# An attention stage rewritten ahead of two feed-forward layers on one core: host-side layout, spans of 38 keys, softmax in PSUM, a new order of stages

## The reference

```python
q_d = q.reshape(B, H, Sd, 4, D).mean(axis=3)      # k_d, v_d likewise; Sd = 144
out_d = sm_attn(q_d, k_d, v_d)                    # full softmax attention over 144 positions
out_up = np.repeat(out_d, 4, axis=2)
mask = np.abs(pos[:, None] - pos[None, :]) < 4    # local attention: 7 keys for each query
scores = np.where(mask, scale * np.matmul(q, k.transpose(0, 1, 3, 2)), -1000000000.0)
attn = softmax(scores); out_local = np.matmul(attn, v)
x = (out_up + out_local) as (B*S, H*D)            # 1152 x 512
h = x @ w_in; x = (h * sigmoid(h)) @ w_out        # w_in 512x2048, w_out 2048x512
p = domain_probs / (domain_probs.sum(-1, keepdims=True) + 1e-09)
out += p[:, e:e+1] * (np.maximum(x @ w1[e], 0.0) @ w2[e])   # 4 experts, each 512x1024x512
```

## Time and profile before

| what | value |
|---|---|
| median of 3 runs | 708.74 us (707.76 to 709.19) |
| the profiled execution: its time, its span | 708.72 us, 706.6 us |
| PE busy | 676.7 us (96%) |
| DVE, ACT, POOL busy | 241.7, 187.9, 173.5 us |
| first score product to the last pair's | 8.0 to 81.2 us |
| first `out1` product | at 103.85 us |

### The profile page before, as it was taken

One profiled execution on the slowest core, in us unless ns is written; L12 is line 12 of the kernel. 1 busy time (PEld: TensorE's weight loads), 2 busy tenths in 40 slices (PEclk: granted clock), 3 DMA queues, 4 the chain that ended last, 5 costly groups with the idle time before them and its releaser, 6 DMA issues.

```text
span 706.6 us, 11146 instructions
## 1 busy us (share of the span) xinstructions
PE 676.7 (96%) x3958; PEld 622.3 (88%) x3958; DVE 241.7 (34%) x376; ACT 187.9 (27%) x399; POOL 173.5 (25%) x121
## 2 busy tenths in 40 slices
PE   6768889999999999999999999999999999999997
PEld 5546679999999999998989899999999998989896
DVE  6988968753222322221221212121212121212211
ACT  4765873322111213343101142111241111101010
POOL 5836467660000004546000063000261000000000
PEclk9986989999999999999999999999999999999999
DMA  9454523430000002324100033000040000001001
GB/s 183 102 107 97 136 77 129 143 116 1 1 1 1 0 0 89 119 90 142 36 0 0 1 120 119 0 0 0 30 148 0 0 0 0 0 0 45 21 23 45
DMA packets 66870, 37.48 MB, mean 53 GB/s; under 512 B 32672, under 2 KB 59552, under 8 KB 66848
## 3 DMA queue, kind: packets, MB, share of 16 engines
q1 hardware_dynamic: 66848, 37.19, 18.7%
HBM read 34.82 MB, written 2.36 MB: 53 GB/s over the span
## 4 chain that ended last, share of the span: by engine, by line
PE 88%; DVE 4%; SPq 3%; issue 2%; DMA 1%; ACT 1%; DVEq 0%; POOL 0%; ACTq 0%; POOLq 0%
PE ps L874 42%; PE ps L940 28%; PE ps L924 14%; SPq L278 2%; DMA k_raw<-k 1%; SPq L258 1%; PE ps L789 1%; PE ps L856 1%; PE ps L777 1%; PE ps L841 1%; DVE g_hi L713 1%; PE ps L885 1%; DVE pl L669 0%; DVE kz L434 0%; DVE mx L643 0%
## 5 line engine op out<-in xcount | busy, mean ns | idle before, releaser
L733 DVE SCALAR_TENSOR_TENSOR g_lo<-ps,g_hi 128x384 fp32r<-128x384 f32 x96 | 53.5, 558 | 270.7 <-ACT g_hi L568 270.7
L568 ACT ACTIVATE g_hi<-ps 128x384 fp32r<-128x384 f32 x96 | 47.1, 491 | 293.5 <-PE ps L874 293.5
L397 POOL TENSOR_TENSOR wa_lo<-w_raw,wa_hi 128x1024 f32 (+1 forms) x24 | 57.4, 2395 | 214.8 <-ACT wa_hi L440 214.8
L874 PE MATMUL ps<-x_hi,wa_hi 128*128 (+1 forms) x288 | 97.6, 339 | 2.2 <-issue 2.2
L874 PE MATMUL ps<-x_hi,wa_lo 128*128 (+1 forms) x288 | 97.4, 338 | 0.0
L874 PE MATMUL ps<-x_lo,wa_hi 128*128 (+1 forms) x288 | 97.2, 338 | 0.0
L874 PE MATMUL ps<-x_hi,wb_hi 128*128 (+1 forms) x288 | 96.9, 336 | 0.0
L874 PE MATMUL ps<-x_lo,wb_hi 128*128 (+1 forms) x288 | 96.9, 336 | 0.0
L874 PE MATMUL ps<-x_hi,wb_lo 128*128 (+1 forms) x288 | 96.8, 336 | 0.0
L397 POOL TENSOR_TENSOR wb_lo<-w_raw,wb_hi 128x1024 f32 x24 | 57.7, 2408 | 106.7 <-ACT wb_hi L440 106.4
L713 DVE CAST g_hi<-g_act 128x384 fp32r<-128x384 f32 x48 | 42.7, 889 | 111.3 <-ACT g_act L563 111.3
(11 more groups left out here) (99 smaller groups left out, 1018.5 us busy)
## 6 DMA issues: line engine op xcount, KB each, us to landing
w_raw<-moe_w SPq DMA_DIRECT2D x64, 256.0 KB, 2.8
w_raw<-moe_w_in SPq DMA_DIRECT2D x16, 256.0 KB, 2.9
w_raw<-moe_w_out SPq DMA_DIRECT2D x16, 256.0 KB, 3.0
q_raw<-q SPq DMA_DIRECT2D x16, 144.0 KB, 3.6
k_raw<-k SPq DMA_DIRECT2D x16, 144.0 KB, 3.7
v_raw<-v SPq DMA_DIRECT2D x8, 288.0 KB
out<-o_acc SPq DMA_DIRECT2D x9, 256.0 KB, 2.0
v_win<-v SPq DMA_DIRECT2D x56, 35.0 KB
```

Source lines behind the costliest of these rows:

```text
L397: pool.tensor_tensor(lo[:, at, :].rearrange("p o n -> p (o n)"), w_raw[:, s, :], hi[:, at, :].rearrange("p o n -> p (o n)").bitcast(F32), ...
L568: act.activation(g_hi[:, f % GB, :], ps[:, HB + f % 4, 0:NB], ACT.Relu).then_inc(relu_done, 1)
L733: dve.scalar_tensor_tensor(out=g_lo[:, f % GB, :], in0=ps[:, HB + f % 4, 0:NB], scalar=0.0, in1=g_hi[:, f % GB, :].bitcast(F32), op0=ALU.m ...
L874: ins = pe.matmul(dst, w[:, f % HALF, c], x[:, kt, at], start=(kt == 0 and i == 0), stop=(kt == KT - 1 and i == 2))
```

## The change

**Layout by the host.** The kernel gets five arrays that the host has only rearranged: qk (for each pair, 128 features by 576 queries and 582 keys, the ends repeated), vw (for each pair, head and group of 32 queries, 48 rows of v), vr (v for the means), w (one contiguous 512 KB block a unit), and the probabilities. SP issues four DMAs a pair (one qk, one v, two windows) where it issued fourteen, and one a weight unit where it issued two. The transposes of q and k and their copies out of PSUM are gone.

**Spans of 38 keys.** GQ goes from 64 to 32 queries, W from 70 to 38 keys: 18 groups. Each head is a product of its own on 64 rows of the array (36 products of 32x38 instead of 9 of 64x140); the scores of a partition are 380 elements instead of 700. The values are 36 products of 64x32 instead of 18 of 64x64, and the probabilities of both heads share a transpose (5 instead of 10).

**Softmax in PSUM.** Mask, maximum, subtraction, exponential and sum work in place on two PSUM banks; only the last multiplication writes SBUF. There is one such pair of banks, so a pair's scores wait until the pair before has been multiplied (`pe.wait_ge(pl_ready, n)`).

**Order of stages.** A pair's scores, softmax and mean softmax are in one step, its transposes one step later, its values two steps later; ten steps in all, written out without a loop, instead of eleven with one. DVE normalises the mean softmax (was ACT), ACT computes its bias (was DVE). ACT does `x_high` and `split_hi` last in a step. x_hi and x_lo of pairs 4 to 7 come after the first weight units. EARLY changes from steps 1, 2, 8, 10 to 1, 2, 3, 8.

```diff
-GQ = 64
+GQ = 32
+HS = 64
+ROWS = 48
-        EARLY = {1: 0, 2: 1, N: 2, N + 2: 3}
+        EARLY = {1: 0, 2: 1, 3: 2, N: 3}
...
+            def load_qk(n):
+                if n >= 2:
+                    sp.wait_ge(s_full, n - 1)
+                    sp.wait_ge(qkd_ready, 2 * n - 2)
+                sp.dma_start(qk_raw[:, n % 2, :], qk[n]).then_inc(qk_in[n % 2], 16)
...
+            def load_win(n):
+                if n >= 2:
+                    sp.wait_ge(pv_done, n - 1)
+                for h in range(2):
+                    sp.dma_start(v_win[HS * h:HS * h + ROWS, n % 2, :, :].rearrange("p g d -> p (g d)"), vw[n, h])\
+                        .then_inc(vw_in[n % 2], 16)
...
# POOL
+            def step(s):
+                stage(s, down_qk)
+                stage(s - 1, down_v)
+                if s - 4 in range(XHALF):
+                    x_low(s - 4)
+                if s in EARLY:
+                    u = EARLY[s]
+                    low_unit(u + 1, slice(u, u + 1), areas[0], u % RAW)
...
# ACT
+            def step(s):
+                if s == N + 1:
                     hidden1(0, 0)
+                stage(s - 2, evac_p1)
+                stage(s - 2, evac_pd)
+                stage(s - 1, evac_p0)
+                stage(s, exp_local)
+                stage(s, exp_down)
...
+                stage(s - 2, evac_up)
+                if s - 4 in range(XHALF):
+                    x_high(s - 4)
+                if s in EARLY:
+                    split_hi(EARLY[s])
...
# DVE
+            def mask_scores(n):
                 dve.wait_ge(s_full, n + 1)
...
+                m = mask[:, :, :].rearrange("p t j -> p (t j)").unsqueeze(1).to_broadcast([P, 2, LC])
+                dve.tensor_tensor(local_scores(0, LC), local_scores(0, LC), m, ALU.add).then_inc(dve_step, 1)
...
+            def norm_down(n):
+                par = n % 2
+                dve.wait_ge(expd_done, 4 * n + 4)
                 dve.tensor_scalar(rsde[:, :], rsd[:, :], EPS, float(R), ALU.add, ALU.mult).then_inc(rsde_done, 1)
...
+                dve.tensor_tensor(pd[:, par, :, :], pd[:, par, :, :],
+                                  rrd[:, :].unsqueeze(2).to_broadcast([HQ, 4, SD]), ALU.mult).then_inc(pd_ready, 1)
...
# PE
+            def scores(n):
+                par = n % 2
+                pe.wait_ge(qk_in[par], 16 * (n // 2 + 1))
+                if n >= 1:
+                    pe.wait_ge(pl_ready, n)
...
+                    for h in range(2):
+                        rows = slice(D * h, D * h + D)
+                        ins = pe.matmul(ps[GQ * c:GQ * c + GQ, SLB + h, at:at + W],
+                                        qk_raw[rows, par, GQ * g:GQ * g + GQ],
+                                        qk_raw[rows, par, S + GQ * g:S + GQ * g + W], start=True, stop=True)
...
+            def values(n):
+                par = n % 2
+                pe.wait_ge(p0_out, n + 1)
+                pe.wait_ge(p1_out, n + 1)
+                pe.wait_ge(vw_in[par], 32 * (n // 2 + 1))
+                if n >= 1:
+                    pe.wait_ge(xf_done, n)
...
+            def step(s):
+                if s == N + 1:
+                    in1(0, 1)
+                stage(s, scores)
...
+                stage(s - 1, turn_p0)
+                stage(s, scores_down)
...
+                stage(s - 2, values)
+                if s == N:
+                    pe.wait_ge(xlo_done, XHALF)
+                    pe.wait_ge(expd_done, 4 * N)
+                    in1(0, 0)
+                stage(s - 1, turn_p1)
```

More of the change, by code:

```diff
@@ L173, in program, with stage, x_of @@
         block = ctx.enter_context(nc.Block())
[L181 to L205, removed]
-        EARLY = {1: 0, 2: 1, N: 2, N + 2: 3}
[L210 to L229, removed]
+        def stage(n, do):
+            if 0 <= n < N:
+                do(n)
+        EARLY = {1: 0, 2: 1, 3: 2, N: 3}
+        XHALF = N // 2
+        def x_of(x, n):
+            return x[:, n % KT, (n // KT) * S:(n // KT) * S + S]
         def tile1(blk, f):
@@ L301, in _ @@
+            load_qk(0)
+            for s in range(N + 1):
+                step(s)
+            with sp.Fori(2, (FT1 + E * FT2) // RAW) as i:
                 for s in range(RAW):
@@ L574, in end1 @@
                     copy(x_hi[:, j, bass.ds(blk * NB, NB)], ps[:, ACCB + j, 0:NB]).then_inc(x2hi_done, 1)
-            steps(act, step, 4)
+            act.wait_ge(band_set, 2)
+            for c in range(2):
+                copy(*window_mask(c)).then_inc(mask_set, 1)
+            for s in range(N + 2):
+                step(s)
             AHEAD = len(EARLY)
@@ L710, in hidden1, with step @@
+            def step(s):
+                stage(s, mask_scores)
+                stage(s, max_local)
+                stage(s, sub_max)
+                stage(s, max_down)
+                stage(s, norm_local)
+                stage(s, norm_down)
+                stage(s - 2, final)
+                if s == N:
+                    hidden1(0, 0)
             def hidden1(t, f):
@@ L716, in hidden1 @@
                                   ALU.subtract).then_inc(g_ready, 1)
-            steps(dve, step, 3)
+            dve.wait_ge(band_set, 2)
+            for c in range(2, QP):
+                dve.tensor_copy(*window_mask(c)).then_inc(mask_set, 1)
+            down_k(0)
+            for s in range(N + 2):
+                step(s)
             dve.wait_ge(pr_in, 16)
@@ L819, in scores, with warm, turn_local @@
-            def scores(duo, par):
-                for bank in range(2):
-                    pe.wait_ge(tp_free[bank], tp_before_qk(duo, par) + 2)
-                if late(duo, par, 1):
-                    pe.wait_ge(masked, 2 * pair(duo, par))
+            def warm(count):
+                for _ in range(count):
+                    pe.transpose(ps[:, OUTB, 0:P], ident[:, :], ident[:, :])
+            def turn_local(n, bank, at, t):
+                return pe.transpose(ps[0:PW, TB + bank, at:at + P],
+                                    pl[:, n % 2, t, :, :].rearrange("p h j -> p (h j)")[:, 0:PW], ident[:, :])
@@ L833, in scores, with scores_down @@
                 ins.then_inc(s_full, 1)
-            def scores_down(duo, par):
-                pe.wait_ge(qkd_ready, 2 * pair(duo, par) + 2)
-                if late(duo, par, 1):
-                    pe.wait_ge(expd_done, 4 * pair(duo, par))
+            def scores_down(n):
+                pe.wait_ge(qkd_ready, 2 * n + 2)
+                if n >= 1:
+                    pe.wait_ge(expd_done, 4 * n)
                 for half in range(2):
-                    ins = pe.matmul(ps[0:HQ, SDB + half, 0:2 * SD], qd[:, half * HQ:(half + 1) * HQ],
-                                    kd[:, :, :], start=True, stop=True)
+                    for h in range(2):
+                        rows = slice(D * h, D * h + D)
+                        ins = pe.matmul(ps[0:HQ, SDB + h, half * SD:half * SD + SD],
+                                        qd[rows, half * HQ:half * HQ + HQ], kd[rows, :], start=True, stop=True)
```

666 lines of the change are left out of this document (282 added, 384 removed).

## The result

The changed kernel takes 711.88 us (median of 20 runs, 710.04 to 712.62) where the kernel before takes 708.29 us beside it. The ratio is 1.0046, interval [1.0031, 1.0061]: slower by about half a per cent, where 692 was forecast. The profiled execution took 711.14 us with a span of 709.3 (before 708.72 and 706.6).

What follows compares the result with a forecast made beforehand. PE bounds the kernel, so only the second matrix's start moves: first steps to 21.7 us, loops to 75.2, end 85.4, clock 87.5; against 103.85 that takes 16.35 us off 708.7, giving 692 (own range 686 to 699, widened to 681 to 705).

Steps and rivals of the forecast that it cites:

- the loop through POOL: Attention steps: POOL's means, PE's mean scores and values, ACT's split, POOL's lo part; 9.85 us with a weight unit, 8.45 with x.
- the 2.1 us for the clock: Attention part: allowance for some half-clock PE work, 2.1 us in all, moving the second matrix's start from 85.4 to 87.5.
- The first load and step: Start of attention: q loaded at 4.7 us, scores done at 7.1, first weight unit's lo part done at 21.7.
- DVE, SP, DMA: Attention steps: DVE 6.3 us a step at 0.55 per PSUM operation, SP's 7.54 us gone, DMA free behind the first load.
- The wait for kd: Sign of being right: PE waits for POOL's kd before mean scores, POOL never idle between x_lo and the next sum of q.
- Its tests of size: Signs of being right: 9 to 10 us between pairs' scores at first, 8 to 9 in steps 4 to 7; out1 at 80 to 94.
- Its sign of being wrong: PE in attention: 72 narrow instructions taking well under 1.8 or over 3 us.
- the full-clock row for narrow products: PE's local scores and values: 0.031 us an instruction, 2.2 us for 72, with bounds of 1.1 and 4.4 us.
- Rival 3: Half clock throughout attention, or a stall of 1 to 3 us at weight unit 8: start at 99, time 703; chance 0.13.
- The wait of 0.95: Feed-forward layers: PE's 0.95 us wait ahead of 111.29, shortly after the second matrix starts, expected to remain.
- rival 1: PE's narrow products overlap on the two row halves, 1.1 us per 72: time 683.5; chance 0.2.
- rival 2: PE's narrow products are slow, 0.061 us each, 4.4 us per 72: time 716; chance 0.10.

Runs made afterwards that it cites:

- e9: The changed kernel with ACT doing x_high and split_hi ahead of its copies and exponentials, as before the change: 696.17 us, ratio 0.9808.
- e3: The changed kernel with POOL's four late x_lo put one behind each of weight units 4 to 7: 709.27 us, ratio 1.0024.
- e1: The changed kernel with POOL forming the next pair's q and k means before x_lo or the weight unit's lo part: 694.84 us, ratio 0.9834.
- e4: The changed kernel with local values using 32 of 64 features of v as weights, half the result left out: 697.38 us (1 run).
- e2: The changed kernel plus six unused identity products on PE ahead of the mean scores of steps 1 to 7: 700.64 us, ratio 0.9899.
- e8: The changed kernel plus twelve unused transposes on PE ahead of the mean scores of steps 1 to 7: 696.2 us (1 run).
- e7: The changed kernel with the edits of e1 and e3, plus six unused identity products a step on PE: 691.85 us, ratio 0.9778.
- e11: The changed kernel with the edits of e1 and e3, plus three unused identity products a step on PE: 694.90 us, ratio 0.9797.
- e6: The changed kernel with the edits of e1 and e3 together: 689.54 us, ratio 0.9753.

## Why the prediction was wrong

The forecast was 692; the time went to 711.9, outside the range. The mechanism that it put first, the loop through POOL, is there. One term of the sum, the 2.1 us for the clock, was far too small: about 17 us were due. A stall in the layers, which it had only in a rival, came on top.

- **The first load and step: 2.55 us better.** The first scores start at 4.21 us (4.7 forecast), the lo part of unit 0 ends at 19.15 instead of 21.7: 2.55 us gained. The 72 score instructions take 1.08 us, not 2.2, so one term was mis-sized by half in the helpful direction.
- **DVE, SP, DMA: right.** DVE's PSUM operations take 0.55 to 0.56 us at any time, as assumed; the 7.54 us of SP's queue and PE's wait for q are gone, and nothing waits for a transfer in the steps.
- **The loop: right in its links.** In the step above: means 2.34 (2.35 forecast), up to the start of x_lo 0.93 (1.0), x_lo 1.37 (1.44). The wait for kd, POOL without idle time between x_lo and the next q: as stated. Its tests of size failed: 11.07 us in steps 4 to 7 where 8 to 9 was named, and out1 at 102.53 where 80 to 94 was. Its sign of being wrong, 72 narrow instructions well under 1.8 or over 3 us, came both ways: scores 1.08, values 4.05.
- **The clock: the step that failed.** "PE waits 1 to 2.5 us in every loop, so I expect some of it, and add 2.1 us in all: 87.5." The prediction itself gave a loop's growth as 1.1 us "and more if the narrow products double as well". They double: mean scores 1.17 for 0.7, values with mean values 5.26 for 2.95, together 2.8 us a loop, less 0.2 by which the other links were shorter. The six loops took 68.5 us where 53.5 were forecast, so 15.0; in one of them the mean scores ran at full clock. Behind them half clock takes 3.5 more (values with mean values 5.15 us for 2.9, `in1(0, 0)` 3.3 for 2.1), and the values of pair 6 begin another 1.2 late, since four transposes of pair 7 stand ahead of them. Sum: 15.0 + 3.5 + 1.2 - 2.55 = 17.15 against the 2.1 put in: 15 us, which is 102.53 - 87.5. The reason given for the clock, that PE waits in each loop, is not shown: with no wait for kd left, e9 had 0.50 as well.
- **What I read wrongly.** The kernel before showed half clock already, in the very rows used: values 2.19 us for 36 instructions where they take 1.1 at full clock. I took the full-clock row for narrow products "because it is the nearest in shape", and the half-clock row only as the end of the range. But both are rows of the same product, L856, and only the clock differs. The sum should have asked which of the two levels the new step would have. An estimate from the half-clock row, with mean scores and mean values doubled: 2.35 + 1.3 + 5.7 + 0.31 + 0.7 + 1.44 = 11.8 us a loop, near the 11.07 measured. Rival 3 named the clock, but priced it at 1.5 us a loop, where the change shows 2.8; its 12 us are more than six loops at 1.5 give (9), and its start at 99 gives 704, not 703.
- **The layers: wrong by 4.0.** The wait of 0.95 stayed in the sum. It is gone, and one of 1.89 us behind the four x_lo came in its place, with 1.7 us of half clock behind it; `out1(0, 0)` itself ran 1.6 us longer at half clock. The wait is the stall of rival 3, "1 to 3 us". e3 has 3.4 of the 4.0 less, 1.9 by its edit and 1.5 by the clock.
- **Rivals 1 and 2.** Narrow products overlap (rival 1): its price of 0.015 us fits the scores, 0.014 us at half clock and 0.011 at full clock, but not the values. Slow at 0.061 (rival 2): its price was about right for the values, 0.055, but as a matter of the clock, and only for one of the two kinds. The 0.031 at full clock is confirmed at 99.67. The Trainium skill, "TensorE: Matmul & The Clock Gate", section "Wait — 56ns, not 53.3ns?", says that starts never come closer than about 25 ns, however small the product. The scores here do not agree: in e1's timeline 72 of them start within 0.76 us, 10.6 ns each.

```profile
9.76 0.83 PE L708 MATMUL ps<-qk_raw 64*32 64x38 f32 x72 [0.99 <-DVE pl L566]
10.52 0.65 PE L665 MATMUL ps<-ident,pl 128*102 128x128 f32 x4
```

Not settled: why the loads of the scores' 32 weight columns hide and those of the values do not (e4's values with 32 columns still take 0.030 us, twice the scores); and why gapless PE work is granted half clock in one step and 0.74 on average in another, so what sets the clock in these steps.

## What to carry to other kernels

Before pricing a new order, price every PE link of it twice, by rows of each clock level, and where the kernel before shows the lower level in its own steps (0.69 on average in the earlier trace rows) give that sum a real chance. Then look for what closes the loop: here one line of order on POOL, or ACT's place for x_hi and the weight split, was worth 15 to 17 us, while the rewrite as it stood took 42 us of work off DVE and gained nothing. Extra PE work paid here where PE was waiting for POOL (e2, e8), and not where it was not (e7, e11).

## What the runs showed of the hardware

- PE busy for 9.70 of 9.70 us (e9) and 10.00 of 10.00 (e6) was granted 0.50 all the time. A full busy share in the trace was no sign of the high clock.
- Products that nobody reads (e2), and transposes too (e8), raised it: 0.56 to 0.75 and 0.76 over 72 us.
- In the first 13 us of the change the record reads 1.00, yet the mean scores at 6.04 and 11.77 take 1.24 us, as they do at 0.50. There the durations are the safer reading.
- Scores of 64 rows, 32 weight columns and 38 moving ones start 0.014 us apart at half clock (the change, 29.11) and 0.011 at full (e1, 9.76); the values (38 rows, 64 and 32 columns) 0.055 and 0.031.
- DVE's cast of g_hi in SBUF takes 2.43 us at 124.05, while POOL makes wb_lo (123.84 to 128.68), and 0.35 us at 129.02, when POOL is idle. That POOL stretches it is read from this coincidence; no run isolates it.
